# Attention, top-2 experts and a gated output block: 128 rows per tile in attention, and keys and values loaded by plain DMAs and added on POOL

## Chip, cores and metric

The kernel runs on one core of a Trainium2 chip. The metric is the device time of one execution in microseconds. The kernel before takes 1929.85 us, the median of three runs (1929.79 to 1931.75).

## What is computed

```python
# attention: B=8, H=8, S=576, D=64; keys and values averaged over 8 rows: 72 keys
k_p = k.reshape(B, H, 72, 8, D).mean(axis=3);  v_p = likewise
attn = softmax(q @ k_p.T / sqrt(D));           x = (attn @ v_p) as (4608, 512)
# experts: E=8, 512 -> 1024 -> 512, every row goes to the two best
noisy = x @ w_gate + log1p(exp(x @ w_noise)) * noise
out[row] += softmax(top-2 of noisy)[k] * (relu(x[row] @ w1[e]) @ w2[e])
# output block: 512 -> 2048 -> 512
h = out @ w_in;  return (h - tanh(h)) @ w_out
```

All inputs and the result are float32.

## The kernel before

Everything is written out by hand for five queues: SP issues plain DMAs, POOL issues indirect ones (and some plain ones) and does a little arithmetic, PE, ACT and DVE compute. They are tied together by semaphores only; each queue runs in its own order. There are three stages: attention with routing, the experts, the output block. The last two work on blocks of 256 rows with float32 split into a high and a low part, three matmuls for each product (L833 to L835, L842 to L844).

**Attention** is a loop over 8 batches; one pass is a *body* of 8 steps, one step for each head u. The 576 query rows of a head are laid out as 96 partitions of 6 rows each (`TP = 96`, `TT = 6`), so there are 6 tiles of 96 rows. In step s PE computes the scores of head s (`scores`, L708: two tiles of D=64 are stacked to K=128 and multiplied with a block diagonal `kT` of 2x72 columns, so 3 matmuls of 144 columns), transposes q of the next head (L695, 3 transposes), transposes the probabilities of head s-2 (L717, 6 transposes) and multiplies those of head s-3 with the values (L731, 6 matmuls of 81 columns: 64 of x, 16 of gate logits, 1 for the denominator). A float32 matmul that isn't a transpose leaves two records in the profile. ACT takes exponentials tile by tile (L992), and moves `qT` and `pT` from PSUM to SBUF (L979, L984). DVE takes the largest score of each row (`largest`, L1245, 432 columns) and divides by the denominator (`normalise`, L1252 and L1255, 480 columns).

**Keys and values** are summed over groups of 8 rows. The rows of a batch half (`part` 0 or 1, 4 heads) lie on 96 partitions in 3 groups of 8 rows x 64 columns. SP loads the first 4 rows of each group (`load_k`, `load_v`, L323 and L329), then POOL issues a second DMA that *accumulates* the other 4 rows onto them in SBUF (`add_keys`, `add_values`, L502 and L509). DVE halves what is left twice (L1224, L1227, L1236, L1239) and releases the buffer for the load of the next batch. In batch 0 the second halves are loaded plainly into the memory of `x_sb` (`load_late`, `late_rows`) and added by DVE (L1214).

**Routing** of batch b-1 or b-2 is done by DVE in parts 0 to 5 between the steps of body b: sum of the gate logits of 8 heads, log1p, noise, the two largest of 8 experts for each tile (L1308, L1317), the position of each row in its expert's list, with PE counting (L759 to L762, tiles of 48 columns for 6 x 8), weights (`wt`) and slot numbers (`slot_i`). SP stores the slot numbers, loads them back with the two slots of a row apart (`store_slots`, `load_slots`), and POOL writes row numbers to the slots by 9 indirect DMAs of 128 numbers in each batch (`scatter`, L538). Each waits until the last but one has landed. POOL's queue in body b is: keys and values of batch b+1 part 0, last 4 scatters of batch b-3, keys and values of part 1, first 5 scatters of batch b-2. The scattered row numbers themselves come from an iota that goes through a DRAM tensor (`row_all`, `row_flat`, `row_w`) in body 0.

From body 2 on ACT and DVE also split the first expert's weights (`split`, L1060 and L1401), twice in a body and four times in the last.

**SP's queue** in a body: 4 loads of q, 2 of k, 2 of v, 4 stores of x, the slot store and load, 2 stores of `wt`. q of a pair of heads is loaded once PE has transposed the same pair of the batch before.

**Hand-over.** After 5 batches' scatters POOL fetches the rows of two early expert blocks (L562, L569); PE begins on them as soon as the last head is done, at about 235 us. Meanwhile the scatters of batches 5 to 7 go out, and the further blocks need all of them.

## Time and profile before

| | |
|---|---|
| median of three runs | 1929.85 us |
| profiled execution, its own time | 1930.99 us |
| its span | 1929.3 us |
| PE busy | 1886.9 us (98%) |
| DVE busy | 997.1 us (52%) |
| ACT busy | 817.8 us (42%) |
| POOL busy | 518.1 us (27%) |
| DMA packets | 94360, 152.22 MB |

All times in the profile are of one execution and are counted from the start of its span. "Busy" of PE counts pipelined matmuls, whose ends are modelled. A line of a timeline gives start and length; lengths of successive instructions may overlap, so the distance between starts is the better measure of a rate. The granted clock of PE is given as a share of 2.4 GHz.

### The profile page before, as it was taken

How to read it: one execution, taken by the hardware profiler on the slowest of the kernel's cores; microseconds unless marked ns; L12 is line 12 of the kernel's file. 1: busy time of each engine (PE TensorE's matmuls, PEld its weight loads, DVE VectorE, ACT ScalarE, POOL GpSimd, SP SyncE). 2: the span in 40 equal slices, each digit the busy share in tenths (PEclk: the TensorE clock that was granted, in tenths of full speed). 3: DMA queues.
4: the chain of work that ended last, by engine and by line, in shares of the span. 5: the costliest groups of instructions: out<-in, count | busy, mean ns of one | idle time of the engine just before them, and what ended most of it. 6: DMA issues, size and time to landing. Idle time of an engine off the chain costs nothing.

```text
span 1929.3 us, 35482 instructions
## 1 busy us (share of the span) xinstructions
PE 1886.9 (98%) x13064; PEld 1719.3 (89%) x13065; DVE 997.1 (52%) x1920; ACT 817.8 (42%) x1719; POOL 518.1 (27%) x507
## 2 busy tenths in 40 slices
PE   7999899999999999999999999999999999999999
PEld 6988888898999999999989888999999999999998
DVE  5888733413122131312313177666677777776665
ACT  5988623324222232322323254444444444444444
POOL 2254552122111121211122332222322222222222
PEclk9999899999999999999999999999999999999999
DMA  8987534314113141321314120001100000100000
GB/s 194 234 189 166 133 82 142 131 44 150 46 65 109 43 138 47 114 71 45 129 48 143 71 77 34 33 33 50 48 33 33 33 33 33 33 33 33 33 33 22
DMA packets 94360, 152.22 MB, mean 79 GB/s; under 512 B 18912, under 2 KB 62048, under 8 KB 91488
## 3 DMA queue, kind: packets, MB, share of 16 engines
q1 hardware_dynamic: 70304, 100.24, 16.6%
q0 software_dynamic: 24000, 51.26, 9.8%
q8 instruction: 32, 0.52, 0.1%
q14 instruction: 24, 0.20, 0.0%
HBM read 110.54 MB, written 40.40 MB: 78 GB/s over the span
## 4 chain that ended last, share of the span: by engine, by line
PE 88%; DMA 4%; DVE 3%; issue 2%; POOL 2%; ACT 1%; ACTq 0%; DVEq 0%; SPq 0%; POOLq 0%
PE banks L844 14%; PE banks L843 14%; PE banks L842 14%; PE banks L833 13%; PE banks L835 13%; PE banks L834 13%; DMA slot_row<-row_w,slot_w 3%; PE banks L823 3%; POOL slot_row L538 1%; PE banks L708 1%; PE banks L731 1%; POOL k_raw L502 0%; DVE w_lo L1401 0%; PE banks L717 0%; PE banks L869 0%
## 5 line engine op out<-in xcount | busy, mean ns | idle before, releaser
L833 PE MATMUL banks<-x_hi,w_hi 128*128 128x256 f32 x2304 | 637.7, 277 | 6.1 <-DVE x_lo L1420 4.0
L835 PE MATMUL banks<-x_hi,w_lo 128*128 128x256 f32 x2304 | 637.2, 277 | 0.0
L834 PE MATMUL banks<-x_lo,w_hi 128*128 128x256 f32 x2304 | 637.0, 276 | 0.0
L842 PE MATMUL banks<-w_hi,h_hi 128*128 128x512 f32 x1184 | 467.3, 395 | 3.0 <-DVE h_lo L1502 3.0
L844 PE MATMUL banks<-w_hi,h_lo 128*128 128x512 f32 x1184 | 466.0, 394 | 0.0
L843 PE MATMUL banks<-w_lo,h_hi 128*128 128x512 f32 x1184 | 463.1, 391 | 0.0
L833 PEld LDWEIGHTS banks<-x_hi,w_hi 128*128 128x128 f32 x2304 | 433.5, 188 | 9.1 <-DVE x_lo L1420 4.5
L834 PEld LDWEIGHTS banks<-x_lo,w_hi 128*128 128x128 f32 x2304 | 433.3, 188 | 2.5
L835 PEld LDWEIGHTS banks<-x_hi,w_lo 128*128 128x128 f32 x2304 | 433.2, 188 | 0.0
L671 POOL TENSOR_SCALAR large<-u_sq 128x512 uint8<-128x512 f32 x144 | 222.4, 1545 | 568.7 <-ACT u_sq L1153 302.0
L1427 DVE SCALAR_TENSOR_TENSOR h_lo<-banks,h_hi 128x512 fp32r<-128x512 f32 x144 | 99.6, 692 | 362.5 <-ACT h_hi L1082 351.4
L842 PEld LDWEIGHTS banks<-w_hi,h_hi 128*128 128x128 f32 x1184 | 222.5, 188 | 48.2 <-issue 4.1
L844 PEld LDWEIGHTS banks<-w_hi,h_lo 128*128 128x128 f32 x1184 | 222.5, 188 | 47.0
L843 PEld LDWEIGHTS banks<-w_lo,h_hi 128*128 128x128 f32 x1184 | 222.5, 188 | 46.4
L1420 DVE TENSOR_TENSOR x_lo<-banks,x_hi 128x512 fp32r<-128x512 f32 x116 | 74.7, 686 | 253.3 <-ACT x_hi L1075 253.3
L1075 ACT ACTIVATE x_hi<-banks 128x512 fp32r<-128x512 f32 x116 | 63.0, 595 | 300.3 <-PE banks L823 300.3
L1082 ACT ACTIVATE h_hi<-banks 128x512 fp32r<-128x512 f32 x136 | 81.3, 598 | 251.4 <-PE banks L835 251.4
L603 POOL DMA_INDIRECT y<-x_rows,idx_g x76 | 74.1, 975 | 389.6 <-PE banks L823 361.6
L1534 DVE SCALAR_TENSOR_TENSOR g<-u_sq 128x512 f32<-128x512 f32 x144 | 100.3, 696 | 97.8 <-ACT u_sq L1153 97.8
L1155 ACT ACTIVATE th<-banks 128x512 f32<-128x512 f32 x144 | 86.2, 599 | 146.7 <-DVE g L1547 146.7
L1401 DVE TENSOR_TENSOR w_lo<-w_raw,w_hi 128x512 fp32r<-128x512 f32 x160 | 102.3, 685 | 42.1 <-ACT w_hi L1060 42.0
L1547 DVE COPY_PREDICATED g<-large,th 128x512 f32<-128x512 uint8 x144 | 107.2, 744 | 26.7 <-DVE g L1543 26.7
(167 smaller groups left out, 2049.9 us busy)
## 6 DMA issues: line engine op xcount, KB each, us to landing
w_raw<-in_moe_w SPq DMA_DIRECT2D x32, 1024.0 KB, 5.0
y<-y_rows SPq DMA_DIRECT2D x17, 1024.0 KB, 5.2
q_sb<-in_q SPq DMA_DIRECT2D x32, 288.0 KB, 6.3
x_rows<-x_sb SPq DMA_DIRECT2D x32, 288.0 KB, 4.7
out_x<-y_sb SPq DMA_DIRECT2D x36, 256.0 KB, 2.1
k_raw<-in_k SPq DMA_DIRECT2D x16, 288.0 KB, 4.8
v_raw<-in_v SPq DMA_DIRECT2D x16, 288.0 KB, 6.4
w_raw<-in_moe_w_in SPq DMA_DIRECT2D x4, 1024.0 KB, 4.8
```

The source lines that it names most:

```text
L671: pool.tensor_scalar(large[:, :], u_sq[j % 2][:, :], SERIES_MAX ** 2, None, ALU.is_gt).then_inc(large_ready, 1)
L833: pe.matmul(part, hi, x_hi[:, c, :], start=(c == 0), stop=False)
L834: pe.matmul(part, hi, x_lo[:, c, :], start=False, stop=False)
L835: mm = pe.matmul(part, lo, x_hi[:, c, :], start=False, stop=(c == NC - 1))
L842: pe.matmul(p_y[m][:, :], hi, w_hi[par][:, o:o + DM], start=(j == 0), stop=False)
L843: pe.matmul(p_y[m][:, :], hi, w_lo[par][:, o:o + DM], start=False, stop=False)
L844: return pe.matmul(p_y[m][:, :], lo, w_hi[par][:, o:o + DM], start=False, stop=(j == tiles - 1))
L1155: act.activation(th[:, :], p_h[j % PH], ACT.Tanh).then_inc(th_ready, 1)
L1401: dve.tensor_tensor(w_lo[par][:, cols], w_raw[c % 2][:, o:o + 512], w_hi[par][:, cols].bitcast(f32), ALU.subtract).then_inc(split_lo, 1)
L1427: dve.scalar_tensor_tensor(out=pair(h_lo, j), in0=p_h[j % PH], scalar=0.0, in1=pair(h_hi, j).bitcast(f32), op0=ALU.max, op1=ALU.subtract). ...
L1534: dve.scalar_tensor_tensor(out=g, in0=u, scalar=SERIES[0] / SERIES[1], in1=u, op0=ALU.add, op1=ALU.mult).then_inc(poly_ready, 1)
L1547: dve.copy_predicated(g, large[:, :], th[:, :]).then_inc(tanh_done, 1)
```

## The change

The 576 rows of a head become 4 tiles of 128 rows and one of 64 (`TG = 4`, `TH = 64`, `TT = 5`, `ROWS = [128, 128, 128, 128, 64]`). Partition p holds rows 4p to 4p+3 and, for p below 64, row 512+p. Every load or store by rows becomes two DMAs, one for the 512 rows and one for the last 64: q, x, slots, weights of the route (whose two arrays become one), noise. Scores take 2 matmuls of 144 columns and one of 72; values 5 matmuls of 81. Instructions over all tiles run on 128 partitions and 5/6 of the columns. PSUM and SBUF behind the half tile are set once before the start.

Keys and values of every batch are loaded by SP in two plain DMAs, the second halves into new buffers `k_more` and `v_more`. POOL adds them (96x768) where it issued the accumulating DMAs; in batch 0 DVE adds as before. The row numbers come from one iota directly. The layout of `slot_i` and `wt` puts the two slots of a row side by side.

```diff
+    TP = 128
+    TG = S // TP
+    TH = S - TG * TP
+    TT = TG + 1
+    FULL = TG * TP
+    KP, KC = 96, 3
...
             def load_q(b, p):
...
-                sp.dma_start(q_sb[:, p, :, :], q_v[:, bass.ds(b * H + 2 * p, 2), :]).then_inc(q_in[p], 16)
+                u = b * H + 2 * p
+                sp.dma_start(q_sb[:, p, 0:2 * TG * D].rearrange("p (r n) -> p r n", r=2), q_full[:, u:u + 2, :]).then_inc(q_in[p], 16)
+                sp.dma_start(q_sb[0:TH, p, 2 * TG * D:2 * TT * D].rearrange("p (r n) -> p r n", r=2), q_half[:, u:u + 2, :]).then_inc(q_in[p], 16)
+
+            def load_halves(src, raw, more, b, part, done):
+
+                rows = src[:, b * 2 + part:b * 2 + part + 1, :, :].rearrange("p o c n -> p (o c) n")
+                sp.dma_start(raw[:, part, :, :], rows[:, :, 0:CD]).then_inc(done[part], 16)
+                sp.dma_start(more[:, part, :, :], rows[:, :, CD:2 * CD]).then_inc(done[part], 16)
...
             def store_x(b, p):
                 sp.wait_ge(normed, b * H + (2 * p + 2))
...
+                sp.dma_start(x_v[b, 0:FULL, cols].rearrange("(p t) n -> p t n", t=TG), x_sb[:, 0:TG, p, GW:GW + 2 * D]).then_inc(x_out[p], 16)
+                sp.dma_start(x_v[b, FULL:S, cols], x_sb[0:TH, TG, p, GW:GW + 2 * D]).then_inc(x_out[p], 16)
...
             def add_keys(b, part):
 
-                pool.wait_ge(k_in[part], (b + 2) * 16)
-                settle(pool)
-                pool.dma_start(k_raw[:, part, :, :], k_v[:, bass.ds(b * 2 + part, 1), :, CD:2 * CD].rearrange("p o c n -> p (o c) n"),
-                               accum_op=ALU.add).then_inc(k_acc[part], 16)
+                pool.wait_ge(k_in[part], (b + 1) * 32)
+                pool.tensor_tensor(k_raw[:, part, :, :], k_raw[:, part, :, :], k_more[:, part, :, :], ALU.add).then_inc(k_acc[part], 1)
...
-            pool.iota(row_all[:, :, :], pattern=[[2 * S, B], [1, 2], [2, TT]], base=2 * PAD, channel_multiplier=2 * TT
-                      ).then_inc(iotas, 1)
+            pool.iota(row_w[:, :, :], pattern=[[2 * S, B], [1, WAY]], base=2 * PAD, channel_multiplier=WAY).then_inc(iotas, 1)
...
                 wait(pe, exped, b * H + (u - 1))
-                for t in range(HALF):
-                    mm = pe.matmul(p_s[u % 2][0:TP, t * 2 * KEYS:(t + 1) * 2 * KEYS], qT[:, t * TP:(t + 1) * TP],
-                                   kT[:, u, :], start=True, stop=True)
+                for t in range(TG // 2):
+                    pe.matmul(p_s[u % 2][:, t * 2 * KEYS:(t + 1) * 2 * KEYS], qT[:, t * TP:(t + 1) * TP],
+                              kT[:, u, :], start=True, stop=True)
+                r = u % 2
+                mm = pe.matmul(p_s[u % 2][0:TH, TG * KEYS:TT * KEYS], qT[r * D:(r + 1) * D, FULL // 2:FULL // 2 + TH],
+                               kT[r * D:(r + 1) * D, u, r * KEYS:(r + 1) * KEYS], start=True, stop=True)
...
-                for t in range(TT):
-                    i, o = divmod(t, HALF)
-                    mm = pe.matmul(p_o[u % 2][0:TP, t * VW:(t + 1) * VW], pT[u % 4][:, i, o * TP:(o + 1) * TP],
+                for t, n in enumerate(ROWS):
+                    mm = pe.matmul(p_o[u % 2][0:n, t * VW:(t + 1) * VW], pT[u % 4][:, t * TP:t * TP + n],
                                    vp[:, u, :], start=True, stop=True)
...
+            for i in range(2):
+                dve.memset(p_s[i][TH:TP, TG * KEYS:TT * KEYS], 0.0)
+                dve.memset(p_o[i][TH:TP, TG * VW:TT * VW], 1.0)
+            dve.memset(noise_sb[TH:TP, :, TG, :], 0.0)
+            dve.memset(msum[TH:TP, TG, :], 0.0)
...
-                dve.tensor_tensor(msum[:, :, :], m12[:, 0, :, :], m12[:, 1, :, :], ALU.add).then_inc(m_ready, 1)
+                dve.tensor_tensor(msum[:, 0:TG, :], m12[:, 0, 0:TG, :], m12[:, 1, 0:TG, :], ALU.add)
+                dve.tensor_tensor(msum[0:TH, TG, :], m12[0:TH, 0, TG, :], m12[0:TH, 1, TG, :], ALU.add).then_inc(m_ready, 1)
```

## Rows read from the trace of the kernel before

**Rows 1.** Busy time of the attention stage: span, busy us (instructions), PEclk, DMA share, GB/s

```profile
0.00:235.00 235.00, 206.98 (x2009) 196.77 (x2010) 184.00 (x642) 179.67 (x607) 91.47 (x101) 0.97 0.81 187
```

**Rows 2.** The same columns (PE, PEld, DVE, ACT, POOL): body 1, and bodies 2 to 6

```profile
44.58:68.48 23.90, 23.90 (x262) 23.57 (x261) 19.95 (x72) 22.16 (x79) 5.13 (x5) 1.00 0.99 209
68.48:200.72 132.24, 122.85 (x1258) 116.37 (x1257) 114.07 (x419) 110.51 (x380) 58.75 (x56) 0.99 0.84 192
```

**Rows 3.** Waits in bodies 2 to 6: us in total, times, longest

```profile
DVE v_raw L1236 <- DMA v_raw<-in_v: 3.7, 4, 1.4
...
DVE k_raw L1224 <- DMA k_raw<-in_k: 3.0, 2, 2.3
```

**Rows 4.** Timeline of POOL: start, us, in body 4 and near the end of attention

```profile
138.09 1.20 POOL L502 DMA_DIRECT2D k_raw<-in_k  x1
...
140.70 1.09 POOL L538 DMA_INDIRECT slot_row<-row_w,slot_w  x1 [0.30 <-issue]
...
147.52 0.96 POOL L538 DMA_INDIRECT slot_row<-row_w,slot_w  x1 [4.42 <-DMA slot_row<-row_w,slot_w]
...
227.15 1.00 POOL L538 DMA_INDIRECT slot_row<-row_w,slot_w  x1 [0.30 <-issue]
...
230.20 0.97 POOL L538 DMA_INDIRECT slot_row<-row_w,slot_w  x1 [0.77 <-DMA slot_row<-row_w,slot_w]
```

**Rows 5.** DMA queues from 120 to 147 us: packets, MB, share of 16 engines

```profile
q1 hardware_dynamic: 4857, 3.49, 47.7%
q0 software_dynamic: 1504, 1.19, 31.6%
```

**Rows 6.** The chain of waits on PE in body 1, one head: start, us

```profile
62.43 0.74 PE banks L708 x6
63.17 0.25 PE banks L695 x3
63.42 0.49 PE banks L717 x6
63.91 1.01 PE banks L731 x12
```

**Rows 7.** Groups of instructions on DVE up to 235 us: busy us, mean ns

```profile
L1224 DVE TENSOR_TENSOR k_raw<-k_raw 96x384 f32<-96x384 f32 x16 | 8.7, 547 | 3.1 <-DMA k_raw<-in_k 3.0
...
L1227 DVE TENSOR_TENSOR kp<-k_raw 96x192 f32<-96x192 f32 x16 | 5.7, 354 | 0.5
```

**Rows 8.** Groups on POOL over the whole span: its only addition

```profile
L649 POOL TENSOR_TENSOR y<-y,u_sq 128x512 f32<-128x512 f32 x2 | 2.6, 1299 | 0.2
```

**Rows 9.** DMA issues on the page: count, KB each, median us from issue to landing

```profile
k_raw<-in_k POOLq DMA_DIRECT2D x14, 288.0 KB, 6.7
```

**Rows 10.** Timeline of PE in bodies 6 and 7, where its clock is at half

```profile
191.50 1.45 PE L731 MATMUL banks<-vp,pT 128*96 128x81 f32 x12 [2.52 <-DVE x_sb L1255]
...
193.23 1.64 PE L708 MATMUL banks<-kT,qT 128*96 128x144 f32 x6
...
229.94 2.18 PE L731 MATMUL banks<-vp,pT 128*96 128x81 f32 x12 [0.58 <-DVE x_sb L1255]
```

**Rows 11.** Timeline of SP's queue: one issue of a key load in body 4

```profile
121.36 0.60 SPq L323 DMA_DIRECT2D k_raw<-in_k  x1
```

**Rows 12.** Timeline of DVE and POOL in the output stage

```profile
1123.45 1.88 POOL L671 TENSOR_SCALAR large<-u_sq 128x512 uint8<-128x512 f32 x1 [1.65 <-ACT u_sq L1153]
1123.89 1.10 DVE L1534 SCALAR_TENSOR_TENSOR g<-u_sq 128x512 f32<-128x512 f32 x1
...
1127.55 1.50 POOL L671 TENSOR_SCALAR large<-u_sq 128x512 uint8<-128x512 f32 x1 [2.22 <-DVE g L1547]
1128.02 0.70 DVE L1534 SCALAR_TENSOR_TENSOR g<-u_sq 128x512 f32<-128x512 f32 x1
...
1216.34 0.69 DVE L1534 SCALAR_TENSOR_TENSOR g<-u_sq 128x512 f32<-128x512 f32 x1 [5.75 <-ACT u_sq L1153]
1216.43 1.95 POOL L671 TENSOR_SCALAR large<-u_sq 128x512 uint8<-128x512 f32 x1 [17.60 <-ACT u_sq L1153]
```

More of the change, by code:

```diff
@@ L132, in attention_moe_ffn @@
         slot_f = sb("slot_f", [TP, 2, TT], c=a_ctx)
-        slot_n, slot_r, slot_c, slot_i = (sb(n, [TP, 2, TT], i32, c=a_ctx) for n in ("slot_n", "slot_r", "slot_c", "slot_i"))
-        wt = [sb(f"wt{i}", [TP, TT], c=a_ctx) for i in range(2)]
-        row_all = sb("row_all", [TP, B, 2 * TT], i32, c=a_ctx)
+        slot_n, slot_r, slot_c = (sb(n, [TP, 2, TT], i32, c=a_ctx) for n in ("slot_n", "slot_r", "slot_c"))
+        slot_i = sb("slot_i", [TP, TT, 2], i32, c=a_ctx)
+        wt = sb("wt", [TP, TT, 2], c=a_ctx)
         row_w = sb("row_w", [128, B, WAY], i32, c=a_ctx)
@@ L161, in attention_moe_ffn @@
         kT = sb("kT", [128, H, 2 * KEYS], c=a_ctx)
-        qT = sb("qT", [128, HT], c=a_ctx)
+        qT = sb("qT", [128, S // 2 + TH // 2], c=a_ctx)
         vp = sb("vp", [128, H, VW], c=a_ctx)
         pr = [sb(f"pr{i}", [TP, TT * KEYS], c=a_ctx) for i in range(4)]
-        pT = [sb(f"pT{i}", [128, 2, HT], c=a_ctx) for i in range(4)]
+        pT = [sb(f"pT{i}", [128, S], c=a_ctx) for i in range(4)]
         a_ctx.close()
@@ L169, in attention_moe_ffn @@
         w_lo.append(sb("w_lo1", [128, WE], f32r))
-        c_w = [sb(f"c_w{i}", [128, TC]) for i in range(2)]
+        c_w = sb("c_w", [128, TC, 2])
         idx_g = sb("idx_g", [128, SUB], i32)
         idx_s = sb("idx_s", [128, SUB], i32)
-        sb("spacer", [128, 80])
+        sb("spacer", [128, 88])
         x_hi = sb("x_hi", [128, NC, NB], f32r)
@@ L253, in attention_moe_ffn @@
         SPLIT_FIRST, SPLIT_FROM = 7, 3
+        ROWS = [TP] * TG + [TH]
         def is_first(b):
@@ L381, in store_route @@
             def store_route(b):
-                for i in range(2):
-                    sp.dma_start(tw_v[i][:, bass.ds(b, 1), :], wt[i][:, :].rearrange("p (o t) -> p o t", o=1)
-                                 ).then_inc(route_out, 16)
+                sp.dma_start(tw_v[b, 0:FULL, :].rearrange("(p t) i -> p (t i)", t=TG),
+                             wt[:, 0:TG, :].rearrange("p t i -> p (t i)")).then_inc(route_out, 16)
+                sp.dma_start(tw_v[b, FULL:S, :], wt[0:TH, TG, :]).then_inc(route_out, 16)
             def body(b, ahead=False):
@@ L441, in _ @@
             sp.wait_ge(route_out, 32 * B)
-            for i in range(2):
-                sp.dma_start(c_w[i][:, :].rearrange("p (b m) -> p b m", m=SUB),
-                             tok_w[i].rearrange("(b p m) -> p b m", p=128, m=SUB)).then_inc(c_w_in, 16)
+            sp.dma_start(c_w[:, :, :].rearrange("p (b m) i -> p b (m i)", m=SUB),
+                         tok_w.rearrange("(b p m) i -> p b (m i)", p=128, m=SUB)).then_inc(c_w_in, 16)
             def weights(e, nxt, after):
@@ L978, in q_cols @@
                 wait(act, scored, b * H + u)
-                act.activation(qT[:, :], p_q[:, 0:HT], ACT.Copy, scale=SCALE).then_inc(qT_ready, 1)
+                n = FULL // 2 + (TH if u % 2 == 0 else 0)
+                act.activation(qT[:, 0:n], p_q[:, 0:n], ACT.Copy, scale=SCALE).then_inc(qT_ready, 1)
             def probs_cols(b, u):
@@ L989, in exps @@
                 wait(act, p_tr, b * H + (u - 3))
-                for t in range(TT):
+                for t, n in enumerate(ROWS):
                     cols = slice(t * KEYS, (t + 1) * KEYS)
-                    ins = act.activation(pr[u % 4][:, cols], p_s[u % 2][0:TP, cols], ACT.Exp, bias=mx[u % 2][:, t:t + 1])
+                    ins = act.activation(pr[u % 4][0:n, cols], p_s[u % 2][0:n, cols], ACT.Exp, bias=mx[u % 2][0:n, t:t + 1])
                 ins.then_inc(exped, 1)
@@ L1209, in consts_late, with add_late @@
                 dve.wait_ge(casts, 3)
-            def add_late(raw, part, i, landed_in):
+            def add_late(raw, more, part, i, landed_in):
                 dve.wait_ge(landed_in, 32)
-                dve.tensor_tensor(raw[:, part, :, :], raw[:, part, :, :], late_rows[:, i, :, :], ALU.add).then_inc(late_added, 1)
+                dve.tensor_tensor(raw[:, part, :, :], raw[:, part, :, :], more[:, part, :, :], ALU.add).then_inc(late_added, 1)
                 dve.wait_ge(late_added, i + 1)
@@ L1348, in part5 @@
                 step(5, b, ins)
-                wait(dve, slot_out, b * 16)
-                step(5, b, dve.scalar_tensor_tensor(out=slot_i[:, :, :], in0=slot_r[:, :, :], scalar=COLS,
+                wait(dve, slot_out, b * 32)
+                step(5, b, dve.scalar_tensor_tensor(out=slot_i[:, :, :].rearrange("p t i -> p i t"), in0=slot_r[:, :, :], scalar=COLS,
                                                     in1=slot_c[:, :, :], op0=ALU.mult, op1=ALU.add))
@@ L1514, in combine @@
                 if isinstance(v, int) and v == 1:
-                    dve.wait_ge(c_w_in, 32)
+                    dve.wait_ge(c_w_in, 16)
                 dve.wait_ge(y_in, v * 16)
                 for m in range(SUB):
-                    w = [c_w[i][:, bass.ds(v * SUB + m, 1)] for i in range(2)]
+                    w = [c_w[:, bass.ds(v * SUB + m, 1), i] for i in range(2)]
                     dve.tensor_scalar(xg[:, m, :], y2[:, m, 0:DM], w[0], None, ALU.mult).then_inc(comb1, 1)
```

109 lines of the change are left out of this document (47 added, 62 removed).

## The prediction

> **What bounds it now.** I began with the busy table of the attention stage [rows 1]: 235 us of a span of 1929, with PE busy for 207 of them. The change touches no arithmetic of the two stages that follow, so whatever happens is decided before 235 us and then carried through unchanged, unless the hand-over to the experts is held up.
>
> Then the same table by body of the batch loop [rows 2]. I cut at the first halving of the second half of the keys, which the DVE does at the head of every body. Body 1 takes 23.90 us with PE busy for all of it and DVE for 19.95: PE is the bound. Bodies 2 to 6 take 132.24 us, 26.45 each, with DVE busy 22.8 each, ACT 22.1 and PE 24.6 on paper. The work that came in with body 2 is routing and weight splitting, nearly all DVE's. The next view, the waits [rows 3], says what else was paid: DVE stood still 3.0 us for keys and 3.7 us for values, both for accumulating DMAs, six waits in all. So in bodies 2 to 6 DVE is the bound, with PE close behind it, and POOL's queue makes it late.
>
> Why POOL is late is in its timeline [rows 4]. The two accumulating issues take POOL from 138.09 to 140.70, 2.6 us. A scatter waits for the landing of the last but one, and the scatter of 140.70 lets that after the next start only at 147.52, so it took 6.8 us to land, with the accumulating DMAs ahead of it in the same queue. Nearer the end, with hardly any other traffic, the same step goes from 227.15 to 230.20, 3.05 us. The DMA table [rows 5] gives the price of accumulation: in 120 to 147 us the software queue took 31.6% of 16 engines for 1504 packets, 137 engine-us. Four accumulating loads are 1152 of these packets (288 KB in pieces of 1 KB); the rest are scatters. If a scatter's packet takes nothing, an accumulating one takes 119 ns; if it takes the 42 ns of the hardware queue's, 106.
>
> **The change, part by part.** *PE.* In the chain at full clock [rows 6], a head costs 0.74 us for scores, 0.25 for q transposes, 0.49 for probability transposes and 1.01 for values. Scores: six records of 144 columns at 0.123 become four, plus two of 72 columns; for those I take the 0.084 of the values' records: 0.66, a saving of 0.08. Values: 12 records at 0.084 become 10, saving 0.17. Transposes move the same 288 and 576 columns; the half tile counts as a whole short record, so +0.04. Net -0.2 us a head, -1.6 a body. That a weight load 128 wide isn't slower is read from the q transposes, whose weights are already 128 columns and follow each other every 0.083 us.
>
> *DVE.* From 384 and 192 columns [rows 7] a column costs (547-354)/192 = 1.0 ns. The search for the largest shrinks from 432 to 360 columns, the normalising from 480 to 400: 152 ns a head, 1.2 us a body. Routing: one of six index searches and of six maxima goes (0.2 us), some 25 short operations lose 8 or 16 columns (0.3), one is added (0.1): 0.4. Together -1.6 a body. ACT loses one of six exponentials a head, 0.2 us; it is not the bound and I count nothing, since DVE and PE finish later than it in every body.
>
> *Keys and values.* DVE waits for POOL's add now instead of an accumulating DMA. A POOL addition of 128x512 takes 1.30 us [rows 8]; this one has 768 columns, so 1.95 by proportion. Two in a row cost POOL 3.9 us where the issues cost 2.6, +2.6 a body. The data is there 1.95 us after the loads have landed and POOL comes by, where the accumulating DMA took 6.7 us from issue to landing [rows 9]. Hence the 6.7 us of DVE waits should go, and with the longest of them the fall of the clock: after PE's gap of 2.52 us the scores at 193.23 are 1.64 us long [rows 10], against the chain's 0.74 and the little overlap that this view counts with it. With the transposes behind them I take 1 us. POOL's round in a body is four adds (7.8), three landings waited for and three further scatter issues of 1.1; with landings of 4.5 us, between the quiet 3.05 and the loaded 6.8, it is 24.6 us beside a body of some 25, so it stays nearly level with DVE, and its delay of under 8 us is covered by the adds being issued that much ahead of their need.
>
> *SP.* It issues 29 DMAs in a body where it issued 16 (q and x doubled, the other halves of k and v, one slot store more). At the 0.60 us of an issue [rows 11] that is 17.4 us of a 25 us body. Behind them stand loads and stores whose buffers are due a body later, so I cost them at nothing; if that cover failed, eight additional q and x issues of 0.6 would delay a slot list by up to 5 us, and only the scatters behind it. The packets of q rise from 192 to 384 a pair, 768 in a body at 42 ns or less, 32 engine-us; accumulation gives back 1152 x (106 - 42) ns = 74 at least. DMA gets lighter.
>
> *Start, row numbers, output.* Six small memsets of PSUM and tails come before the first keys: each less than the 0.35 us of a 192-column operation [rows 7]; of 0 to 2 us I take 0.4 in all, as they have 81 columns or fewer but for one. The round trip of the row numbers goes from POOL's queue in body 0, where nothing was waiting: nothing. Expert and output stages: nothing, the lists are as long as before.
>
> The sum: start and body 0, -1.6 + 0.4, rounded to -1.1 since its scores run at half clock; body 1, -1.6; bodies 2 to 6, 5 x -1.6 = -8.0; DVE waits -6.7; clock -1.0; body 7 -1.6, and three sets of values at half clock (2.18 us at 229.94, [rows 10]) losing a sixth each, -1.1. Together **-21.1 us**.
>
> *Against it: POOL and DVE reading together.* Before, POOL did no arithmetic in this stage; now it does for 7.8 us a body, just where DVE adds halves and runs routing. The timeline of both engines in the output stage [rows 12] shows what meeting costs. At 1216.34 DVE starts an operation with two inputs from SBUF; POOL's comparison, started 0.09 us later, takes 1.95 us instead of the 1.50 it has elsewhere. In the other order, POOL first by 0.44, DVE's operation took 1.10 us at 1123.89; but at 1128.02, 0.47 us behind POOL, it took 0.70 as usual. So POOL holds something for about 0.45 us of that one-input operation and whoever comes second waits. The new additions read three times as many elements. Bounds: nothing per add, or the whole 1.95 less some 0.5 until DVE next reads twice, 1.45. I take the measured 0.45 once per add: 4 x 0.45 x 5 bodies = +9.0. In body 1 DVE has the slack (19.95 of 23.90), in body 7 there are no adds.
>
> -21.1 + 9.0 = -12.1. From the median of 1929.85 that is 1917.75, so **1918 us**; the profiled execution, 1930.99 with a span of 1929.3, would become 1918.9 and 1917.2.
>
> The Trainium skill, page "SBUF — State Buffer", section "Who interferes with whom", says that a VectorE instruction with two SBUF inputs contends with a GpSimd instruction that reads SBUF, and that the second to issue fully blocks until the first finishes. By that rule the term above would be +29 instead of +9, the second rival's case. The trace agrees that they exclude each other, but the 0.70 us at 1128.02, run inside a POOL operation of 1.50, does not agree that it lasts to the end.
>
> **The rivals.** *No meeting cost.* The adds fall beside PSUM reads. For it: DVE's two longest operations of a head read PSUM. Against: keys and values are halved in the very places where the adds come. -21.1: **1909**.
>
> *POOL holds DVE for nearly a whole addition.* Place: DVE's halving and routing instructions in bodies 2 to 6. Price 1.45 x 20 adds = 29; against -21.1 it is +7.9: **1938**, slower. It decides from 21.1/20 = 1.05 us an add on. For it: three times the elements of the operation that held 0.45, so 1.3 is possible. Against: 1128.02, and DVE has about 3.6 us a body not busy that soak up some of it. About 1 us an add gives **1929**, no difference.
>
> *The scatter chain stays.* Landing times don't fall, since the hardware queue is as full; then POOL's round grows by 2.6 us and bodies 3 to 6 follow it: +10.4, against -1.1 - 1.6 - 1.6 - 2.7 = -7.0: +3.4, **1933**. Against: the long landings stand just behind the accumulating issues.
>
> **How the numbers follow.** Forecast 0.42; no meeting cost 0.22; whole addition 0.17; about 1 us an add 0.11; scatter chain 0.08. A measurement of this kernel can tell 0.2%, 3.9 us, from no change. The first two are faster, with a small part of the fourth: 0.65. Same: most of the fourth and the edge of the third and fifth, 0.14. Slower: 0.21. The range goes from just under the second case to the third: 1907 to 1938. Faster cases alone would lie in 1907 to 1925.
>
> **What would show it.** Bodies 2 to 6 at about 25.1 us each (132.24 - 8.0 - 6.7 - 1.0 + 9.0, over 5) instead of 26.45; no DVE wait for keys or values above 1 us in all; POOL additions of 1.9 to 2.4 us; DVE halvings of 0.55 us and short routing operations stretched in places by 0.4 (over 1 us would be the second rival); scatters landing in 3 to 5 us; values at 0.84 us a head; the expert stage as long as before. I am wrong if PE's values don't get shorter, if additions take over 3 us, or if experts begin no earlier than 235 us.

## The result, and the profile after

The changed kernel takes 2006.01 us (median of 1988.35, 2005.05, 2006.97 and 2026.62) where the kernel before takes 1930.61: **ratio 1.036, 95% interval 1.0293 to 1.0426**, 3.6% slower. The forecast was 1918 us in 1907 to 1938. The profiled execution took 2005.05 us with a span of 2003.3. The changed kernel's single runs spread far more than those of the kernel before (in a later repeat 2007.5 to 2105.4 us against 1942 to 1950), and the ratios are formed without the longest of them, so for it and the kernels near it they give the lower end of the loss.

The busy table of the changed kernel, with the columns of [rows 1] and [rows 2] (span, PE, PEld, DVE, ACT, POOL, PEclk, DMA share, GB/s):

```profile
0.00:235.00 235.00, 218.72 (x1326) 168.15 (x1327) 148.49 (x454) 133.68 (x411) 85.39 (x76) 0.96 0.60 152
...
29.50:87.50 58.00, 58.00 (x241) 44.22 (x241) 18.64 (x41) 22.66 (x71) 12.39 (x8) 1.00 0.40 107
...
174.00:186.00 12.00, 12.00 (x52) 9.42 (x52) 5.60 (x16) 6.08 (x18) 4.61 (x4) 0.50 0.38 93
```

In the 235 us in which attention was finished before, PE gets through 1326 matmuls instead of 2009 and is busy for longer, and DVE for 35 us less [rows 1]. So PE is the bound in this stage, and it has become slower: attention's last values start at 294.77 us instead of 229.94 [rows 10], the first expert matmul at 300.1 instead of 235.6. The second thing to see is PEld: with PE busy for 58.00 us of 58, its weight loads fill only 44.22, where they filled 23.57 of 23.90 in body 1 [rows 2].

The chain of waits on PE at full clock, parts of two heads, the counterpart of [rows 6] (a piece's length here is the distance to the start of the next; L705 and L708 are scores, L691 and L693 q transposes, L717 probability transposes, L729 values, L682 key transposes):

```profile
254.27 0.61 PE banks L717 x5
254.88 1.33 PE banks L729 x10
256.22 0.37 PE banks L682 x3
256.58 0.52 PE banks L705 x4
257.11 0.27 PE banks L708 x2
257.37 0.37 PE banks L691 x2
257.74 0.20 PE banks L693
257.94 0.74 PE banks L717 x5
```

Scores cost 0.79 us instead of 0.74, q transposes 0.37 and 0.57 instead of 0.25, probabilities 0.61 and 0.74 instead of 0.49, values 1.33 for 10 records instead of 1.01 for 12. The mean head is 3.26 us against 2.49: +0.77 where the forecast had -0.2.

And the clock. The timeline of PE has the same ten values at two lengths, 2.46 and 1.40 us:

```profile
75.00 2.46 PE L729 MATMUL banks<-vp,pT 128*128 128x81 f32 x10
...
87.78 1.40 PE L729 MATMUL banks<-vp,pT 128*128 128x81 f32 x10
```

Nine heads from 29.5 to 81.6 us and two from 174.0 to 180.6 run at the long one. For the second stretch the column PEclk says 0.50, the 1.2 GHz level; for the first it has no record of a change yet and still prints 1.00, so the records' lengths have to be read. Before, the values at 27.7 us were long and those at 32.2 full; at the end of attention the last three were long [rows 10].

What was forecast for DVE did come. Its groups of instructions up to 295 us (busy time in us and mean ns, then the idle time ahead of them and what ended it):

```profile
L1259 DVE TENSOR_TENSOR x_sb<-banks,rden 128x400 f32<-128x400 f32 x63 | 36.2, 575 | 2.2
L1249 DVE TENSOR_REDUCE mx<-banks 128x5 f32<-128x360 f32 x64 | 33.9, 530 | 76.0 <-PE banks L708 69.8 <-issue 5.0 <-DVE r_t L1284 0.4
L1406 DVE TENSOR_TENSOR w_lo<-w_raw,w_hi 128x512 fp32r<-128x512 f32 x12 | 16.0, 1333 | 10.8 <-ACT w_hi L1059 10.8
L1240 DVE TENSOR_TENSOR v_raw<-v_raw 96x384 f32<-96x384 f32 x16 | 11.9, 741 | 0.1
```

The search is 530 ns, the normalising 575; the waits for keys and values [rows 3] are gone; DVE now waits for PE, 69.8 us ahead of the searches alone. But the weight split (L1406) has a mean of 1333 ns and the halving of the values (L1240) 741, against 680 and 544 where they are undisturbed. The timeline of both engines shows why:

```profile
162.31 4.34 DVE L1406 TENSOR_TENSOR w_lo<-w_raw,w_hi 128x512 fp32r<-128x512 f32 x1 [1.35 <-ACT w_hi L1059]
162.52 1.82 POOL L505 TENSOR_TENSOR k_raw<-k_raw,k_more 96x768 f32<-96x768 f32 x1
164.29 1.81 POOL L510 TENSOR_TENSOR v_raw<-v_raw,v_more 96x768 f32<-96x768 f32 x1
```

A DVE instruction of 0.68 us takes 4.34, until the second of two additions ends. Over the 28 additions I summed how far each DVE instruction that overlaps one exceeds the lower quartile of its own kind: 24.5 us. How much of that PE's slowness covers, no run shows directly; experiment 5 comes back to it.

**Where 74 us of span went.** 64.5 by the start of the experts, made up roughly so: the 11 long heads take 71.1 us, at the 3.73 us of the other 52 they would take 41.0, so the clock is 30.1; 63 head periods of 3.73 instead of 3.21 are 32.8; the start is 1.8 later. The 3.21 is the mean distance of the heads before, with their four at half clock and the bodies in which DVE, not PE, set the pace; so it rises by 0.52 where PE's own head costs 0.77 more. The remaining 9.5 come after it, part of them two further stretches at half clock, from 295.9 and 350.6 us.

### The profile page after: what moved, and what is told of

The parts are those of the page before. It is cut to its first block, busy times and chain, and to the rows that moved or that the text cites. A ratio compares the mean times of both kernels' runs of the same rounds, so it can differ in the third digit from the quotient of the medians.

```text
span 2003.3 us, 35015 instructions
## 1 busy us (share of the span) xinstructions
PE 1965.2 (98%) x12832; PEld 1743.5 (87%) x12833; DVE 1009.9 (50%) x1910; ACT 815.3 (41%) x1655; POOL 535.2 (27%) x505
## 4 chain that ended last, share of the span: by engine, by line
PE 94%; DVE 3%; ACT 1%; issue 1%; DMA 0%; ACTq 0%; DVEq 0%
PE banks L842 13%; PE banks L841 13%; PE banks L840 13%; PE banks L831 13%; PE banks L833 13%; PE banks L832 13%; PE banks L729 4%; PE banks L821 3%; PE banks L717 2%; PE banks L705 2%; PE banks L691 1%; PE banks L708 1%; PE banks L748 1%; DVE w_lo L1406 0%; PE banks L867 0%
## 5 line engine op out<-in xcount | busy, mean ns | idle before, releaser
L1406 DVE TENSOR_TENSOR w_lo<-w_raw,w_hi 128x512 fp32r<-128x512 f32 x160 | 110.4, 736 | 50.9 <-ACT w_hi L1059 50.8
```

Source lines behind the costliest of these rows:

```text
L1406: dve.tensor_tensor(w_lo[par][:, cols], w_raw[c % 2][:, o:o + 512], w_hi[par][:, cols].bitcast(f32), ALU.subtract).then_inc(split_lo, 1)
```

## The experiments

They ran on other chips, where the kernel before took 1930 to 1948 us. Each is compared with the kernel before on its own chip.

**1. One part of the change alone.** Plain loads and POOL's additions on the 96-row layout:

```diff
-                pool.dma_start(k_raw[:, part, :, :], ..., accum_op=ALU.add).then_inc(k_acc[part], 16)
+                pool.tensor_tensor(k_raw[:, part, :, :], k_raw[:, part, :, :], k_more[:, part, :, :], ALU.add).then_inc(k_acc[part], 1)
```

> The kernel before with its 96 row layout, and only the second part of the change: all rows of keys and values by plain DMAs into two tiles each, POOL adding the halves. Theory 1 (the layout makes the kernel slower: the profile of the changed kernel has value matmuls of 128 columns at 0.111 us a record against 0.085 for 96 before, and gaps of 0.1 to 0.2 us on PE where a full tile is followed by the half one and back): this run stays near before, 1915 to 1940 us, the waits of DVE for the keys and the values (6.7 us before) gone, PE's period per head at full clock still 2.74 us. Theory 2 (POOL's adds meet DVE's instructions and the plain loads come too late): near the changed kernel, 1990 to 2005 us, with DVE busy for longer than PE in a body.

Measured: 1972.85 against 1947.55 us, **1.0145 (1.0103 to 1.0186)**. Neither expectation, but between them: some two fifths of the loss are here. The other part, the 128-row layout with accumulating DMAs (the same lines the other way round):

> The changed kernel with its 128 partition layout, but with the accumulating DMAs again for every batch after the first. Theory 1 (layout): it stays slow, 1995 to 2015 us, values' records of 0.111 us and about 3.8 us a head at full clock. Theory 2 (POOL's adds): it comes back to about 1930 us, 1900 to 1940. If both parts share the loss, a time between.

Measured: **1.0268 (1.0214 to 1.0322)**, theory 1, with single runs of 1992.7 to 2144.2 us. The profiled one is the longest: its values, L734 there, are long for the whole of attention, on the page's list of groups (the lower line is the changed kernel's):

```profile
L734 PE MATMUL banks<-vp,pT 128*128 128x81 f32 (+1 forms) x640 | 157.3, 416 | 0.6 <-ACT vp L1007 0.6
```

```profile
L729 PE MATMUL banks<-vp,pT 128*128 128x81 f32 (+1 forms) x640 | 101.4, 302 | 3.6 <-DVE x_sb L1259 3.0 <-ACT vp L1002 0.6
```

So both parts lose by themselves. Their sum is 4.1%, the whole change's 3.6%; by the intervals that difference is none.

**2. What in the layout.** The half tile padded with zeros to a full one on PE, the rest of the change as it is:

```diff
-                for t, n in enumerate(ROWS):
-                    mm = pe.matmul(p_o[u % 2][0:n, t * VW:(t + 1) * VW], pT[u % 4][:, t * TP:t * TP + n],
+                for t in range(TT):
+                    mm = pe.matmul(p_o[u % 2][:, t * VW:(t + 1) * VW], pT[u % 4][:, t * TP:(t + 1) * TP],
```

and the same for scores, q and probabilities.

> The changed kernel with its half tile padded to a full tile of 128 rows and 128 columns on PE, so that no PE instruction of a head changes the tile's shape: 5 value records a pair instead of mixed ones, the same count of matmuls. The padding is zero and goes nowhere. Theory 1 (about 7 gaps of 0.1 to 0.2 us a head at changes of shape): PE's period per head at full clock falls from 3.76 us to 2.7 to 3.0 us, the gaps ahead of the transposes and values of the half tile are gone, and the kernel takes 1925 to 1955 us; if the clock also comes up near 32 us as before, the lower end. Theory 2 (POOL's adds), or a loss by the width of the weights alone: it stays within 10 us of the changed kernel, 1995 to 2015 us.

Measured: **1.0095 (1.0063 to 1.0126)**, all runs within 1961 to 1972 us. More arithmetic, and three quarters of the loss gone. The time is between the two expectations, the period at full clock (2.87 us) as the first had it; the additions are still in it.

Only the width of the weights, on the kernel before (`pT[..., t * TP:t * TP + 128]` in place of 96 columns):

> The kernel before, with the value matmuls' weights taken 128 columns wide instead of 96 (the last 32 are of the next tile, and their result rows are not used); nothing else. If a weight load of 128 columns takes the time of the record (0.111 us against 0.085), ten records a head cost 0.27 us more: 31 to 32 heads of full clock and the rest at half clock give 8 to 20 us, 1938 to 1950 us, with value records of 0.11 us. If the width is free and 0.111 came from something else of the new layout: within 3 us of 1930.6, records of 0.085 us.

Measured: **1.0026 (1.0012 to 1.004)**, 5 us. The timeline of PE, the values and what follows them:

```profile
61.92 1.49 PE L730 MATMUL banks<-vp,pT 128*128 128x81 f32 x12
63.25 0.91 PE L708 MATMUL banks<-kT,qT 128*96 128x144 f32 x6
```

From start to start 1.33 us for 12 records, 0.111 each; with 96 columns 1.01, 0.084 [rows 6]. So the width costs 0.027 us a record, as the first theory had it, but the 5 us are under its 8 to 20: 64 x 0.3 would be 19 us, and PE isn't the bound in every body.

**3. The padded layout without POOL's additions** (experiment 2 with accumulating DMAs):

> The padded kernel of before (128 partitions, the half tile padded to 128 rows and columns on PE) with the accumulating DMAs again after the first batch: the layout without its tile switches and without POOL's adds. Theory A (each POOL add holds every DVE instruction with two operands in SBUF until it ends: 32 us of stretched DVE instructions over 28 adds in the run with POOL's adds alone): DVE has no stretched instruction, PE's period at full clock stays 2.85 us a head, and the kernel comes to within 10 us of the kernel before of the same chip, 1940 to 1957 where before takes 1947, against 1970 with the adds. Theory B (what is left of the loss is the layout's own): it stays at 1960 to 1975.

Measured: 1942.65 against 1947.93 us, **0.9978 (0.9961 to 0.9995)**. This is 0.2% faster than the kernel before, just outside the noise, and 2.9% faster than the same kernel with its half tile (1.0268). One head of its timeline at full clock:

```profile
102.12 0.34 PE L713 MATMUL banks<-kT,qT 128*128 128x72 f32 x2
102.29 0.38 PE L696 MATMUL banks<-ident,q_sb 128*128 128x128 f32 x2
102.51 0.71 PE L722 MATMUL banks<-ident,pr 128*72 128x128 f32 x5
103.06 1.24 PE L734 MATMUL banks<-vp,pT 128*128 128x81 f32 x10
104.14 0.69 PE L710 MATMUL banks<-kT,qT 128*128 128x144 f32 x4
104.67 0.34 PE L713 MATMUL banks<-kT,qT 128*128 128x72 f32 x2
```

A head of 2.55 us. Ten values take 1.08 from start to start, where the changed kernel's ten, two of them on half the columns, take 1.33; the two half scores 0.17 instead of 0.27. Less is computed there and more time passes. (Padding takes away the changes of shape and most of the time at half clock together, so the 2.9% are the worth of both.)

**4. What in the additions.** First plain loads with POOL adding a single element:

> The 96 row kernel with all rows by plain DMAs, POOL adding one element in place of each whole add (so the halves of most rows aren't added, and the output is of other keys and values; the first batch is whole). Theory A (POOL's adds hold DVE, the loads are harmless): the 25 us of the run with the adds go, no DVE instruction stretched, 1930 to 1948 us where before takes 1947, attention ending 10 to 25 us earlier than with the adds. Theory C (the plain loads themselves are late or take DMA time from the outputs): it stays above 1960 us, with DVE waiting for keys and values.

Measured: **0.9986 (0.9973 to 1.0)**; theory A. (The kernel leaves the second half of most rows out of the sums, so its result is another one.) The loads alone gain 3 us, if anything, and the 28 additions cost 1.59% of 1947, 31 us, **1.1 us each**; by the two intervals it is 22 to 39 us. It is the whole price, with what follows from a late DVE: from 28 us to the first expert matmul PE stands still for 30.6 us against 13.0 without the additions, at a mean granted clock of 0.91 against 0.97. In the trace of experiment 1 it looks like this:

```profile
96.98 1.82 POOL L498 TENSOR_TENSOR k_raw<-k_raw,k_more 96x768 f32<-96x768 f32 x1
...
97.55 0.65 DVE L1248 TENSOR_TENSOR x_sb<-banks,rden 96x480 f32<-96x480 f32 x1
98.12 2.85 DVE L1217 TENSOR_TENSOR k_raw<-k_raw 96x384 f32<-96x384 f32 x1
98.75 1.80 POOL L503 TENSOR_TENSOR v_raw<-v_raw,v_more 96x768 f32<-96x768 f32 x1
...
157.82 4.25 DVE L1303 TENSOR_TENSOR diff<-r_mx 96x6 f32<-96x6 f32 x1
158.46 1.82 POOL L498 TENSOR_TENSOR k_raw<-k_raw,k_more 96x768 f32<-96x768 f32 x1
160.23 1.80 POOL L503 TENSOR_TENSOR v_raw<-v_raw,v_more 96x768 f32<-96x768 f32 x1
...
205.34 1.84 POOL L498 TENSOR_TENSOR k_raw<-k_raw,k_more 96x768 f32<-96x768 f32 x1 [6.30 <-DMA k_more<-in_k]
205.53 1.67 DVE L1339 TENSOR_SCALAR slot_r<-slot_n 96x12 int32<-96x12 int32 x1
```

The normalising, which reads PSUM (L1248), keeps its length beside the addition. The halving, both inputs in SBUF, is held until the second addition has ended, 2.85 us instead of 0.54. The subtraction of 6 columns takes 4.25 us instead of 0.17. By its record it even starts 0.64 us before the first addition, while POOL still issues a scatter (157.49 to 158.44); in the two traces of this and of the changed kernel six instructions begin so and are held. Two inputs in SBUF are not needed: the last row has one, and a constant, and takes 1.67 us instead of 0.17. Two additions in a row hold as one in seven of eight such pairs; in the eighth DVE is let in between them. The excess over all 28 is 32.2 us. Then DVE adding by itself:

> The 96 row kernel with all rows by plain DMAs, and DVE itself adding the halves, 4 adds of 96x768 a body, as it does in the first batch. By the 384 column add of 0.55 us, an add of 768 takes about 1.06 us, 28 of them 30 us of DVE, against 32 us of stretched DVE instructions when POOL adds. Theory A (a POOL add costs DVE what it holds): about the same time as with POOL's adds, 1960 to 1980 us where before takes 1947. Theory C (POOL's add is cheap for DVE and something else costs): clearly slower than with POOL's adds, above 1985.

Measured: **1.0087 (1.0054 to 1.012)**. 28 additions of 0.95 us on DVE are 26.5 us of its time. That is about the time of the kernel with POOL's, 8 us less by the medians; the intervals overlap a little, so that it is cheaper is likely and not shown. Then the additions in eight pieces:

```diff
+                for i in range(8):
+                    r, m = (k_raw[:, part, :, i * CD // 8:(i + 1) * CD // 8], k_more[:, part, :, i * CD // 8:(i + 1) * CD // 8])
+                    pool.tensor_tensor(r, r, m, ALU.add).then_inc(k_acc[part], 1)
```

> The 96 row kernel with plain DMAs, each of POOL's adds cut into 8 instructions of 96x96. Theory A1 (POOL holds the shared access until an instruction's end, and lets DVE in between two of them): no DVE instruction is stretched by more than about 0.4 us, the sum of the stretches falls from 32 us to under 12 us, and the kernel comes to 1935 to 1958 us where before takes 1947. Theory A2 (DVE is held as long as POOL has adds to do, or the two share by time): the stretches stay 25 us or more, and the kernel stays at 1965 us or above.

Measured: **0.9995 (0.9979 to 1.0011)**, though POOL is busy with them for 88 us instead of 51. The excess of DVE's instructions falls to 14.3 us. Mostly they are let in between two pieces (the 0.20 and 0.19 of the routing become 0.30 and 0.33), but once one was not, for eleven pieces:

```profile
198.68 0.30 DVE L1287 TENSOR_TENSOR r_yy<-r_y 96x48 f32<-96x48 f32 x1
...
199.34 0.33 DVE L1289 SCALAR_TENSOR_TENSOR r_acc<-r_acc,r_yy 96x48 f32<-96x48 f32 x1
```

```profile
45.38 2.45 POOL L500 TENSOR_TENSOR k_raw<-k_raw,k_more 96x96 f32<-96x96 f32 x7
...
46.20 4.11 DVE L1221 TENSOR_TENSOR k_raw<-k_raw 96x384 f32<-96x384 f32 x1
47.79 3.22 POOL L507 TENSOR_TENSOR v_raw<-v_raw,v_more 96x96 f32<-96x96 f32 x8
```

So the time came back as A1 said, but its bound of 0.4 us an instruction and 12 us in all did not hold.

**5. Both repairs, and one of them.** Padded and in eighths:

> Both repairs on the whole change: 128 partitions with the half tile padded, plain DMAs for all rows, and POOL's adds cut into 8. Theory A (the loss has two causes, the tile switches on PE and the adds that hold DVE, and nothing else): it comes to 1935 to 1946 us where before takes 1947, that is ratio 0.993 to 0.999, no worse than padded with accumulating DMAs (0.998); DVE waits for keys and values gone. If there is a third cause that needs both parts together: above 1955.

Measured: **1.004 (1.0025 to 1.0056)**, better than padded with whole additions (1.0095), worse than padded with the accumulating DMAs (0.9978), and outside theory A's 0.993 to 0.999. There is no large third cause, but of these last 0.6%, 12 us, the cause isn't shown. What the trace has is DVE waiting 14.8 us for POOL's pieces, 9.2 for keys and 5.6 for values, where with the accumulating DMAs it waits 9.7 for these. The changed kernel with its additions in eighths:

> The changed kernel with its tile switches, POOL's adds cut into 8 and nothing else. Theory A: PE is the bound and covers most of what DVE loses, so the ratio to before stays 1.02 to 1.035 (the change alone has 1.036, the layout with accumulating DMAs 1.027), PE's period at full clock 3.5 to 3.8 us a head. Against it: a ratio under 1.01 would mean that the switches cost little once DVE isn't held.

Measured: **1.0176 (1.0142 to 1.0211)**, single runs 1972.3 to 2146.0 us, the longest being the profiled one, at half clock for all of attention. The ratio is just under what theory A gave, its interval reaches it. It is also 1.8% under the changed kernel's 1.036, so PE's slowness doesn't seem to hide all that the additions cost DVE; but of five runs the median is 2005.8 us, and with such a spread the 1.8% can be the clock's as well. Padding the changed kernel's values alone:

> The changed kernel with only the value matmuls' half tile padded to 128 columns; the half tiles of probabilities, scores and queries stay. At full clock the two narrow records of a head (0.205 and 0.12 us) become 0.112 each and the next group loses 0.06 us: theory A gives 0.15 to 0.2 us a head less of 3.76, about 3.6, some 10 to 12 us over 64 heads if the clock stays as in the changed kernel (ratio 1.025 to 1.035 against 1.036); if the clock at the start comes up earlier than at 87.8 us, more. If one switch a head made the whole loss, it would come to the padded kernel's 1.0095.

Measured: 2070.6 to 2131.4 us, the median 2115. All of it is longer than either theory had it. The period at full clock is the 3.6 us of theory A, but only 14 of the heads run at it; the busy table at half clock:

```profile
240.00:300.00 60.00, 60.00 (x261) 47.73 (x259) 27.55 (x94) 25.58 (x78) 18.53 (x14) 0.50 0.38 98
```

**6. Changes of shape in the 96-row kernel.** One of six value tiles 64 columns wide, then every second one (the kernels leave those rows of the output out, so their results are others):

```diff
+                    n = 64 if t == TT - 1 else TP
-                    mm = pe.matmul(p_o[u % 2][0:TP, t * VW:(t + 1) * VW], pT[u % 4][:, i, o * TP:(o + 1) * TP],
+                    mm = pe.matmul(p_o[u % 2][0:n, t * VW:(t + 1) * VW], pT[u % 4][:, i, o * TP:o * TP + n],
```

> The kernel before (96 rows) with the last tile of the value matmuls taken 64 columns of weights wide in place of 96; rows 64 to 95 of that tile of the output are not computed. PE has less to load, and one switch of the tile's shape down and one up a head. By the changed kernel's trace a record just behind a switch starts 0.09 us later than in the run of its shape, and the next group 0.06 us later: theory A gives a gap of 0.17 to 0.21 us ahead of the two narrow records, 0.1 to 0.25 us more a head, 64 heads, 5 to 15 us, ratio 1.002 to 1.010. If the width of 64 alone is harmless in this layout and the gaps come from something else of the 128 layout: records of 0.06 to 0.085 us with no gap, ratio 0.997 to 1.001.

Measured: **1.0017 (1.0004 to 1.0031)**, between the 1.002 to 1.010 of the first expectation and the 1.001 of the second, so the time doesn't decide. The timeline does:

```profile
202.16 1.28 PE L732 MATMUL banks<-vp,pT 128*96 128x81 f32 x12
203.38 0.77 PE L751 MATMUL banks<-wg,vT 64*72 64x80 f32 x8
```

1.22 us from start to start for 12 records of which two have less to load, instead of 1.01. The record behind the change starts 0.18 us after the one ahead of it, the full ones 0.085 apart.

> The kernel before (96 rows) with the second, fourth and sixth tile of the value matmuls 64 columns of weights wide in place of 96, so 6 changes of the tile's shape a head in this group; rows 64 to 95 of those tiles of the output are not computed. With one narrow tile the period at full clock went from 2.74 to 2.97 us, so theory A gives 2.74 + 3 x 0.23 = 3.4 us a head where PE is the bound. Theory C1 (the shape changes alone also hold the clock down): PE stays at half clock well past the 32 us of before, for 8 heads or more in all, and the ratio is 1.02 or more, with a spread of single runs over 20 us. Theory C2 (the clock needs the rest of the 128 layout): it rises by 40 us as before, ratio 1.008 to 1.018 with a spread under 12 us.

Measured: **1.0165 (1.0134 to 1.0196)**, single runs 1976 to 1990 us. The values of two heads, and two stretches of the busy table:

```profile
205.35 1.82 PE L732 MATMUL banks<-vp,pT 128*96 128x81 f32 x12
207.11 0.44 PE L742 MATMUL banks<-ident,vk 96*64 96x96 f32 x3
...
208.86 1.82 PE L732 MATMUL banks<-vp,pT 128*96 128x81 f32 x12
```

```profile
40.00:80.00 40.00, 40.00 (x344) 33.88 (x343) 25.03 (x82) 31.97 (x105) 7.15 (x7) 1.00 0.84 183
...
222.90:250.20 27.30, 23.96 (x119) 20.29 (x120) 10.96 (x46) 12.58 (x40) 2.59 (x4) 0.50 0.33 100
```

Values cost 1.76 us instead of 1.01, 0.25 for each narrow tile, and the period is 3.5. **A change to a narrow matmul tile and back costs PE in this layout too, with less to load.** But not every change of shape does. The kernel before has 128*96, 96*128 and 96*72 in each head, and key transposes of 96*64, and they follow each other without such a gap, here with 1.01 and 0.25 us from start to start (12 and 3 records):

```profile
61.01 1.17 PE L731 MATMUL banks<-vp,pT 128*96 128x81 f32 x12
62.02 0.41 PE L687 MATMUL banks<-ident,kp 96*64 96x96 f32 x3
62.27 0.90 PE L708 MATMUL banks<-kT,qT 128*96 128x144 f32 x6
```

What costs in these traces is a tile of 64 rows, or 64 columns in a matmul that isn't a transpose.

The clock comes up at 35.2 us, near the 32 of the kernel before, and stays full to 222.9, with PE busy for 40.00 of 40 in the first stretch shown. Then it is at half for 27.3 us, four more heads, where the kernel before has 10.2 us from 223.0 on. That is fewer than the 8 heads of C1 and near C2; the spread of 13 us is between the two. In this profile, then, changes of width alone don't bring the long time at half clock at the start; whether they lengthen the later one, it can't say.

**7. The clock.** The changed kernel itself again, and reordered so that half tiles are neighbours:

> The changed kernel itself once more, on the chip of the experiments: how its time spreads, against which the kernels near it are read. In its first profile the granted clock of PE is half until 87.8 us; in two kernels near it the whole of attention ran at half clock in the profiled run and took 2144 and 2146 us. Theory C (the clock is the second half of the loss, and which way it goes is no property of the one kernel): single runs between 1985 and 2150 us, with a spread over 20 us. Against it (the clock goes the same way in every run of a kernel): all runs within 10 us of 2010.

Measured: 1.0358 (1.0319 to 1.0397), single runs 2007.5 to 2105.4 us. Theory C: one and the same kernel spreads by 98 us. Its six runs have a median of 2048.9 us against 1947.4, 5.2% more, where the ratio has 3.6. In this profile the clock came up at 61.6 us instead of 87.8, and was half again for two heads from 223 us and from 250.6 to the end:

```profile
252.00:300.00 48.00, 48.00 (x204) 36.56 (x203) 19.73 (x78) 20.86 (x67) 1.96 (x2) 0.50 0.26 78
```

> The changed kernel with its PE instructions of a head in another order and nothing else: the half tile of the queries comes ahead of the full ones, and the half tile of the values ahead of the full ones, so that the half tiles of scores and queries, and of probabilities and values, are neighbours. 4 changes of the tile's shape a head in place of 7 on the mean. Theory A (each change costs 0.13 to 0.16 us of PE): PE's period at full clock falls from 3.76 us to 3.2 to 3.45 us a head, 20 to 30 us of the whole, ratio 1.010 to 1.028, and the clock is at half no longer than in the changed kernel. If the narrow tiles cost by themselves wherever they stand: the period stays above 3.6 us and the time that of the changed kernel.

Measured: 1.036 (1.0329 to 1.0391), the changed kernel's time. Its period at full clock fell from 3.8 to 3.55 us, less than theory A had. The chain shows that a neighbour of the same kind doesn't help:

```profile
250.96 0.61 PE banks L717 x5
251.57 1.33 PE banks L729 x10
```

The values are still 1.33: behind the half transposes, 64 rows high, the half values, 128 rows high and 64 wide, are another shape. How much the gain at full clock was worth stays open: the profiled execution has 16 heads at half clock, the changed kernel's two have 11 and 19. Last, one kind of half tile at a time, the others padded, with POOL's additions:

> The padded kernel of before (128 partitions, POOL's adds), with the value matmuls' half tile 64 columns wide again: one narrow pair a head, all tiles of scores, queries and probabilities full. Period at full clock 2.87 + 0.16 to 0.26, about 3.05 to 3.15 us a head. Theory R (tiles of 64 rows hold the clock, columns don't): at half clock for no more heads than padded (6 of 62), 1975 to 1990 us, ratio 1.011 to 1.022 against 1.0095 padded. Theory S (any change of shape in this layout does): half clock for 15 heads or more, above 2000 us.

Measured: **1.0164 (1.0147 to 1.0181)**, 1956.5 to 1963.2 us, period 3.08 us, at half clock for 2 of the heads. In the ratio, theory R, as far as one profile tells the heads.

> The changed kernel with the half tiles of probabilities and values padded, those of scores and queries left at 64 rows. Period at full clock about 3.3 us a head. Theory R (tiles of 64 rows hold the clock): half clock for 10 heads or more and a spread of single runs over 20 us, 1990 to 2110 us. Against it: half for fewer than 8 heads, the spread under 15 us, 1975 to 1995 us.

Measured: **1.0213 (1.0186 to 1.024)**, 1966.2 to 1981.9 us, period 3.35 us, half clock for 8 heads. Between the two expectations. So the heads at half clock are more when tiles of 64 rows come in, in single profiles of kernels that spread; what does it, and why padding the values alone made it worst, stays open.

## Why the prediction was wrong

**The step that failed is PE's, -0.2 us a head.** It measured +0.77. Two mistakes are in it. "That a weight load 128 wide isn't slower" was read from the q transposes; the values' records with weights of 128 columns are 0.111 us apart against 0.084 (experiment 2). A transpose doesn't tell that price: those of the probabilities in experiment 3 have weights of 72 columns and are 0.11 apart too, with 128 columns moved, where before 96 moved ones took 0.083. And the half tile was given the price of a short record, +0.04 for all transposes and 0.084 for each half score. A head has seven changes to a half tile or back on the mean. Padded, without them, it is 2.6 us with key transposes left out, so they make about 0.65 of the 3.26, some 0.1 us each; experiment 6 has 0.25 for two. A row that shows one stood in the trace of before:

```profile
69.33 1.17 PE L731 MATMUL banks<-vp,pT 128*96 128x81 f32 x12
70.43 0.77 PE L750 MATMUL banks<-wg,vT 64*72 64x80 f32 x8
```

The gate's matmuls of 64 rows start 1.10 us after the values instead of 1.01, 0.18 behind the last of them, and the first score behind the gate starts 0.16 us after its last record and the second 0.20 after the first, instead of 0.12; the forecast looked at no such record.

The Trainium skill has this as a rule, page "TensorEngine Tiling (Array Packing)", section "Key Properties": "Changing tiling mode (not just tile) drains the TensorE". The gaps at half tiles agree with it. It should have been a rival in the forecast and wasn't, nor was any case in which PE gets slower: this is the larger part of the miss. It isn't all of it: the additions alone, on the old layout, took 1.0145, which on 1930 us is 28 us and past the range's upper end as well.

**The clock, -1.0.** It was costed as the end of one stall. It became +30 us in the profiled execution, at the start of attention above all, and runs of one kernel near it lie 150 us apart (1992.7 and 2144.2). No step asked what would happen to the granted clock if PE's work itself changed.

**Port meeting, +9.0 for 20 additions, 0.45 each.** Mechanism right, size wrong; the case of "about 1 us an add", given 0.11, had the price. Measured on the old layout, 28 additions cost 31 us, 1.1 each with what follows from them (experiment 4), up to 4.1 us for one instruction that meets two. That a pair of back-to-back additions can hold DVE as one was in no case. The 0.45 came from a POOL operation with one input [rows 12], where this one has two, and from a single meeting: in the whole output stage DVE's operation starts behind POOL's 127 times and is held in that one, 1123.89, alone; 17 times it starts first and POOL is held.

The same page that the forecast drew on, the Trainium skill's "SBUF — State Buffer", section "Who interferes with whom", lets the second to issue block until the first has finished. The 2.85 us above agree, and go beyond it: the held instruction outlasted the following addition too. The 4.25 us agree in length, but there DVE's record starts first, so these traces don't confirm the order.

**Key and value waits, -6.7.** They went, as forecast. What they were worth is another matter: the plain loads alone gave 3 us (experiment 4). **POOL's additions**, 1.95 us each: 1.83. **DVE, -1.6 a body**: search 530 and normalising 575 ns for 599 and 654, right, and of no use while PE is the bound. **DMA, SP, row numbers** were costed at nothing, and no wait of theirs shows; SP's doubled issues are in the padded kernel too, which is no slower than before. **The scatter chain** didn't decide: it would have held DVE, and DVE waited for PE (69.8 us ahead of the searches). **Start, +0.4**: the first values are 1.8 us later. **Expert and output stages**: unchanged work, but 9.5 us more from the first expert matmul on, of which only the two stretches at half clock are seen; what else is in it stays open.

The forecast's gain was to come from the layout and the vanished waits. The layout's true gain is small: with full tiles only and the old way of adding it is 0.9978.

## What to carry to other kernels

Before a layout gets an odd tile, look in the trace for the gap ahead of a matmul with a tile of 64 rows or columns: padding to the full shape can be cheaper than computing less. Before an addition is given to an idle POOL, see what DVE does beside it: what read PSUM kept its length here, elementwise work from SBUF to SBUF was held. A whole addition can cost as much as if DVE did it itself, and cut into short instructions much less. Where PE is the bound, read the lengths of its records at the start of the stage, since the clock column may not show that it is at half.

## What was not expected of the hardware

Busy PE does not mean full clock: in experiment 5 it was granted 0.50 for 60 us in which PE was busy for 60.00, and the repeated changed kernel's single runs differ by 98 us. A record of 64 columns behind one of 96 starts 0.18 us later, though it loads a third less. And a DVE instruction of 6 columns that lasts 0.17 us took 4.25.
